# Two downs ahead of the next up at MLP group boundaries, routing two chunks earlier, and no wait behind each of the last slot writes

## The chip, the cores and the metric

The kernel runs on one core of a Trainium2 chip. The metric is the device time of one execution in microseconds, lower is better. Five engines take part: PE (TensorE, the matmuls), DVE (VectorE), ACT (ScalarE), POOL (GpSimd) and SP (SyncE, which only issues DMAs here). Each runs its own instruction list in order, and they meet only at semaphores.

## The reference, cut to what matters

```
scores = scale * q @ k.T, masked to a window of 64      # 4 batches, 8 heads, 576 x 64
x = softmax(scores) @ v                                 # becomes 2304 tokens x 512
h = x @ w_in                                            # 512 -> 2048
x = (h * sigmoid(1.702 * h)) @ w_out                    # 2048 -> 512, the MLP
noisy = x @ w_gate + log1p(exp(x @ w_noise)) * noise    # 8 experts
top2 experts per token, weights = softmax of their two logits
for each expert e: out[tokens of e] += weight * (relu(x @ w1[e]) @ w2[e])   # 512 -> 1024 -> 512
```

## The kernel before, in words

Every fp32 product is made of three fp32r matmuls (high x high, low x high, high x low), so each operand is first split into a high part (ACT, sometimes POOL) and a low part (the rest, by a subtraction on DVE or POOL).

There are three stages: the attention; the MLP; the expert stage, in which tokens lie sorted by expert in a DRAM tensor `x_by_expert` and are worked off in slot tiles of 128 rows.

**The MLP** handles 6 groups (g) of 384 tokens. A group has 16 chunks (c) of the hidden size. On PE an *up* (L1209, 12 matmuls of 384 columns) makes the hidden values of a chunk, and a *down* (L1224, 9 matmuls of 512 columns) adds the chunk to the three accumulators of the group. The down of a chunk stands two places behind its up: up(c), down(c-2). At a group's boundary the order on PE is therefore up(15), down(13), up(0) of the next group, down(14), up(1), down(15), up(2), down(0).

- Between them stand, per chunk: the sigmoid (ACT, L736), its product with the hidden values (DVE, L982), the high part (ACT, L700, `high_of_gate`) and the low part (DVE, L900, `low_of_gate`). In loop step c the two engines do sigmoid and product of chunk c and high and low part of chunk c-1.
- `split_x` makes the high and low parts of the next group's input: four copies on ACT (L695) and four subtractions on DVE (L895). It can start when up(15) has ended, since there is one buffer `xs`. up(0) needs it.
- `copy_y` takes the finished accumulators of a group into `x2` (ACT, L707, two tiles; DVE, L907, one). down(0) of the next group needs the accumulators free. There is one `x2`, so `copy_y` of group g also waits until the scatter of group g-1 has landed:

```
act.wait_ge(accumulated, g * FC + FC)
after(act, x2_turned, g * GT)
after(act, x2_scattered, g * KT * 16)
```

- Routing of group g is threaded through the chunks of group g+1: `turn_x2` and `logits` on PE, `soften`, `choose`, `assign`, `weigh`, `place` on DVE. `place` (last line L967) gives the rows to which tokens go, and then POOL can issue `scatter_x2(g)`, six indirect DMAs (L560) from `x2` to `x_by_expert`.

**POOL during the MLP** splits the expert weights: 128 jobs of two instructions each (L530 high part, L532 low part). Four jobs are a *quad*, so there are 32 quads. SP loads the raw weights and stores both parts. POOL's order is written out by hand: QUADS quads, then for each of the groups 1 to 5 GQUADS quads followed by the scatter of the group before. With QUADS = 2, GQUADS is 6. POOL takes its list in order, so a scatter never starts ahead of the quads in front of it, and a quad never ahead of a scatter that waits.

**The expert stage** takes two ups and a down of 24 matmuls each per slot tile (L1308, L1319: `expert_up` of a tile, then `expert_down` of the tile before). Behind it DVE adds the weighted result to the rows so far (`finish`, L1079), which POOL has gathered from `out` (L599, `gather_part`), and POOL scatters the sum to `out` (L606, `scatter_y`). A gather waits for the writes of earlier experts through a table `settled`; rows of one expert are all different. Tiles from number 35 on are written out one by one, and each of these first waits for its own write before POOL goes on (L634, L640). In this profile 40 tiles run, numbers 0 to 39, and number 35 is the last whose gather waits for an earlier expert.

Of the kernel before, what the change touches and what calls it, by code (L numbers as in the profile page):

```python
# [6 lines left out]
I32 = mybir.dt.int32  # L7
ALU = mybir.AluOpType
# [3 lines left out]
P = 128  # L12
# [28 lines left out]
QUADS = 2  # L41
# [10 lines left out]
FAR = 1 << 16  # L52
LG = 2 * E
# [9 lines left out]
def build(nc, q, k, v, w_in, w_out, w_gate, w_noise, noise, w1, w2, out):  # L63
# [13 lines left out]
    with ctx:  # L77
# [73 lines left out]
        count_to = sbc("count_to", [P, SLOTS])  # L151
        slot_row = sbc("slot_row", [P, SLOTS])
        upto = sbc("upto", [P, E, E], mybir.dt.bfloat16)
        odd = sbc("odd", [P, SLOTS + 1])
# [11 lines left out]
        expert_of = sbc("expert_of", [P, SLOTS], I32)  # L166
        row_of = sbc("row_of", [P, SLOTS], I32)
        ends = sbc("ends", [P, E], I32)
        rows = sbc("rows", [P, SLOTS], I32)
        slot_w = sbc("slot_w", [P, SLOTS])  # L170
        keep = sbc("keep", [P, SLOTS], I32)
        far = sbc("far", [P, SLOTS], I32)
        masked_id = sbc("masked_id", [P, SLOTS], I32)
        passed = sbc("passed", [P, SLOTS, E])
        stepped = sbc("stepped", [P, SLOTS, E])
        past = sbc("past", [P, SLOTS])
        row_f = sbc("row_f", [P, SLOTS])
        first_row = sbc("first_row", [P, SLOTS])
        first_slot = sbc("first_slot", [P, SLOTS])
        settled = sbc("settled", [P, SLOTS], I32)  # L180
        end_row = sbc("end_row", [P, SLOTS])
        valid = sbc("valid", [P, SLOTS])
# [294 lines left out]
        def _(pool):  # L477
# [97 lines left out]
            nc.gpsimd.iota(count_to[:], [[1, SLOTS]], base=0, channel_multiplier=0, allow_small_or_imprecise_dtypes=True).then_inc(slot_consts, 1)  # L575
            nc.gpsimd.iota(slot_row[:], [[P, SLOTS]], base=P, channel_multiplier=0, allow_small_or_imprecise_dtypes=True).then_inc(slot_consts, 1)
            nc.gpsimd.iota(odd[:].rearrange("p (a b) -> p a b", b=2), [[0, (SLOTS + 1) // 2], [1, 2]], base=0, channel_multiplier=0, allow_small_or_imprecise_dtypes=True).then_inc(slot_consts, 1)
# [50 lines left out]
            for j in range(SURE - 1, SLOTS):  # L628
                par = j % 2
                if j < SURE:  # L630
                    gather_part(j, par)
                    scatter_y(j, par)
                    for i in range(2):
                        pool.wait_ge(y_scattered[i], SURE // 2 * 16)  # L634
                else:
                    with pool.If(tiles1 > j + 1):
                        gather_part(j, par)
                        scatter_y(j, par)

                        pool.wait_ge(y_scattered[par], (j // 2 + 1) * 16)  # L640

        @block.scalar
        def _(act):
# [83 lines left out]
            def mlp(g, first):  # L727
                split_x(g)
# [644 lines left out]
```

## Time and profile before

| | us |
|---|---|
| median of 3 runs (lowest, highest) | 1124.26 (1120.97, 1127.78) |
| time of the profiled execution | 1117.89 |
| its span, from first to last instruction | 1116.2 |
| PE busy | 998.9, 89% of the span |
| POOL busy | 528.3, 47% |
| MLP, first up to the end of the last down | 164.0 to 597.8 |
| expert stage, first up to the end of the last down | 642.8 to 1098.5 |

In a timeline a row gives start, length, engine, source line, operation, output and inputs, and in square brackets how long the engine had been idle before it and what ended that. Matmuls of one block are merged into one row; the length of such a row overlaps the next by some 0.16 us, so a block is best measured from its start to the start of the next. A clock of 1.00 is TensorE at 2.4 GHz, 0.50 at 1.2 GHz.

### The profile page before, as it was taken

To read this page: it belongs to the slowest core of one execution; us is meant where nothing else is said; L and a number is where in the kernel's file an instruction comes from. 1 tells how busy PE (TensorE), PEld (TensorE's weight loads), DVE (VectorE), ACT (ScalarE), POOL (GpSimd) and SP (SyncE) were. 2 spreads that over 40 slices of the span, in tenths; PEclk is the share of its full clock that TensorE was granted. 3 is DMA by queue.
4 is the path that set the end of the run, shared out by engine and by line. 5 is a ranking of instruction groups with operands and counts; after the bars stand their busy time and mean duration, and the time that the engine had idled before them with its cause. 6 is when DMAs were issued, how large, how long until landed. Compare 5 with 4: busy or idle time off the path is not lost.

```text
span 1116.2 us, 21003 instructions
## 1 busy us (share of the span) xinstructions
PE 998.9 (89%) x5376; PEld 851.4 (76%) x5377; DVE 628.7 (56%) x1413; ACT 448.6 (40%) x1088; POOL 528.3 (47%) x511
## 2 busy tenths in 40 slices
PE   5777769999999999999996099999999999999993
PEld 5666659879899898898995078888887888888882
DVE  3777752342433527437353467676767676767671
ACT  4877762222424324233242034343443434343440
POOL 3555553896198889898985202121212121212121
PEclk8999989999999999999997599999999999999997
DMA  7678748998189799898888884586858585859211
GB/s 159 166 186 188 184 118 299 289 292 265 40 262 284 253 287 292 270 295 287 265 269 290 279 260 141 183 252 179 255 168 252 169 258 170 266 166 268 65 58 33
DMA packets 253444, 241.65 MB, mean 216 GB/s; under 512 B 97740, under 2 KB 171468, under 8 KB 253392
## 3 DMA queue, kind: packets, MB, share of 16 engines
q1 hardware_dynamic: 215312, 201.54, 60.4%
q0 software_dynamic: 9280, 28.62, 7.2%
q10 hardware_dynamic: 28800, 10.83, 4.3%
q8 instruction: 29, 0.48, 0.2%
q14 instruction: 23, 0.19, 0.1%
HBM read 148.81 MB, written 94.21 MB: 218 GB/s over the span
## 4 chain that ended last, share of the span: by engine, by line
PE 33%; DMA 17%; issue 13%; DVE 11%; ACT 9%; POOL 7%; ACTq 5%; DVEq 2%; POOLq 1%; SPq 1%
PE bank L1209 14%; PE bank L1224 13%; DMA part<-out,yrow 10%; ACT hq L783 4%; DMA out<-y_sb,yrow 4%; ACTq L766 3%; POOL raw L532 2%; ACT he L790 2%; POOL xT L530 2%; DVE y_sb L1079 2%; DMA w_raw<-moe_w_out 1%; PE bank L1244 1%; DVE hT L1067 1%; PE bank L1146 1%; DVEq L1041 1%
## 5 line engine op out<-in xcount | busy, mean ns | idle before, releaser
L1308 PE MATMUL bank<-W,xe 128*128 x960 | 233.2, 399 | 23.5 <-DVE xe L1054 23.5
L1319 PE MATMUL bank<-W,he 128*128 x960 | 230.5, 395 | 4.1 <-DVE he L1071 4.1
L1308 PEld LDWEIGHTS bank<-W,xe 128*128 128x128 f32 x960 | 182.1, 190 | 67.9 <-issue 23.6
L1209 PE MATMUL bank<-xs,W 128*128 128x384 f32 x1152 | 219.8, 340 | 8.7 <-DVE xs L895 8.6
L1224 PE MATMUL bank<-W,gs 128*128 128x512 f32 x864 | 217.1, 396 | 1.0 <-DVE gs L900 1.0
L1319 PEld LDWEIGHTS bank<-W,he 128*128 128x128 f32 x960 | 179.9, 188 | 49.0 <-issue 5.8
L1209 PEld LDWEIGHTS bank<-xs,W 128*128 128x128 f32 x1152 | 200.3, 189 | 17.0 <-issue 10.3
L1224 PEld LDWEIGHTS bank<-W,gs 128*128 128x128 f32 x864 | 161.7, 188 | 31.9 <-DVE gs L900 1.4
L982 DVE TENSOR_TENSOR gate<-bank,gate 128x384 f32<-128x384 f32 x96 | 53.4, 557 | 232.6 <-ACT gate L736 226.2
L606 POOL DMA_INDIRECT out<-y_sb,yrow x40 | 40.6, 1015 | 291.5 <-DVE y_sb L1079 286.1
L783 ACT ACTIVATE hq<-bank 32x256 f32<-32x256 f32 x320 | 119.7, 374 | 112.7 <-issue 99.9
L736 ACT ACTIVATE gate<-bank 128x384 f32<-128x384 f32 x96 | 47.2, 492 | 281.6 <-PE bank L1209 275.0
L1065 DVE STREAM_TRANSPOSE hT<-bank 32x256 f32<-32x256 f32 x320 | 144.0, 450 | 11.2 <-PE bank L1308 6.2
L532 POOL TENSOR_TENSOR raw<-raw,xT 128x512 fp32r<-128x512 f32 x96 | 129.7, 1351 | 7.5
L530 POOL TENSOR_TENSOR xT<-raw,e_iota 128x512 fp32r<-128x512 f32 x96 | 107.0, 1115 | 38.4 <-DMA raw<-moe_w 37.1
L900 DVE TENSOR_TENSOR gs<-gate,gs 128x384 fp32r<-128x384 f32 x96 | 85.1, 888 | 0.0
L773 ACT ACTIVATE xe<-xr 128x512 fp32r<-128x512 f32 x40 | 25.3, 632 | 139.4 <-DVE xr L1050 136.7
L509 POOL TENSOR_TENSOR prob<-prob,rden 128x384 f32<-128x384 f32 x48 | 39.8, 829 | 74.2 <-DVE rden L852 74.2
L1071 DVE SCALAR_TENSOR_TENSOR he<-hT,he 128x1024 fp32r<-128x1024 f32 x40 | 49.0, 1226 | 45.1 <-ACT he L790 45.1
L661 ACT ACTIVATE prob<-prob,nmx 128x128 f32<-128x128 f32 x144 | 56.1, 391 | 27.8 <-DVE nmx L845 27.6
L560 POOL DMA_INDIRECT x_by_expert<-x,xT x36 | 36.9, 1024 | 58.0 <-issue 37.5
L599 POOL DMA_INDIRECT part<-out,yrow x40 | 42.0, 1050 | 34.9 <-POOL yrow L596 34.9
(148 smaller groups left out, 1031.8 us busy)
## 6 DMA issues: line engine op xcount, KB each, us to landing
W<-split_weights SPq DMA_DIRECT2D x128, 512.0 KB
raw<-moe_w SPq DMA_DIRECT2D x128, 256.0 KB, 3.4
split_weights<-raw SPq DMA_DIRECT2D x128, 256.0 KB, 3.3
split_weights<-xT SPq DMA_DIRECT2D x96, 256.0 KB, 3.1
xg<-x_by_expert ACTq DMA_DIRECT2D x160, 64.0 KB
split_weights<-high SPq DMA_DIRECT2D x32, 256.0 KB
q_raw<-q SPq DMA_DIRECT2D x32, 144.0 KB, 2.9
k_raw<-k SPq DMA_DIRECT2D x32, 144.0 KB, 3.9
```

Of the source, the lines that this page charges most:

```text
L530: nc.gpsimd.tensor_tensor(high[buf], job_raw[buf], one, ALU.mult).then_inc(ej_high, 1)
L532: nc.gpsimd.tensor_tensor(job_raw[buf].bitcast(F32R), job_raw[buf], high[buf].bitcast(F32), ALU.subtract).then_inc(ej_low, 1)
L661: ins = nc.scalar.activation(prob[m % 3][:, b], prob[m % 3][:, b], ACT.Exp, bias=nmx[:, m % 2, b:b + 1], accum_out=den[:, m % 2, b:b + 1])
L783: ins = nc.scalar.activation(hq[c * Q:(c + 1) * Q, :].rearrange("p (k q i) -> p k q i", q=2, i=Q)[:, :, q], src[q * Q:(q + 1) * Q, :, c], ...
L900: nc.vector.tensor_tensor(gs[c % 2][:, 1], gate[c % 2][:], gs[c % 2][:, 0].bitcast(F32), ALU.subtract).then_inc(g_low, 1)
L982: nc.vector.tensor_tensor(gate[c % 2][:], h_ps[c % 2][:, 0:TG], gate[c % 2][:], ALU.mult).then_inc(gated, 1)
L1065: nc.vector.transpose(dst[c * Q:(c + 1) * Q, :, q], src[q * Q:(q + 1) * Q, :, c])
L1071: nc.vector.scalar_tensor_tensor(out=he[par][:, 1], in0=hT[:], scalar=0.0, in1=he[par][:, 0].bitcast(F32), op0=ALU.max, op1=ALU.subtract). ...
L1209: ins = nc.tensor.matmul(h_ps[c % 2][:, 0:TG], w_in_s[:, wl, d, c * P:(c + 1) * P], xs[:, xl, d], start=(d == 0 and wl + xl == 0), stop=(d ...
L1224: ins = nc.tensor.matmul(y_ps[t][:], gs[c % 2][:, gl, t * P:(t + 1) * P], w_out_s[:, wl, c], start=(c == 0 and gl + wl == 0), stop=(c == F ...
L1308: ins = nc.tensor.matmul(h2_ps[par][:, f * 512:(f + 1) * 512], xe[par][:, xl, d * P:(d + 1) * P], weights(e, wl, d * FE + f * 512), start= ...
L1319: ins = nc.tensor.matmul(ye_ps[par][:], he[par][:, hl, c * P:(c + 1) * P], weights(e, wl, W1COLS + c * DM), start=(c == 0 and wl + hl == 0 ...
```

## The change

Four things change.

1. At the five group boundaries PE has two downs between up(15) and the next up(0), and two ups behind down(15). ACT and DVE make the parts of chunk 15 right behind `split_x` instead of in step 0.
2. All routing of the group before stands earlier: the copies of the accumulators in step 1 instead of 2, everything after it two steps earlier (`place` in step 12 instead of 14).
3. QUADS is 7 instead of 2, so GQUADS is 5 instead of 6. Ahead of the first scatter POOL has 12 quads instead of 8; ahead of the second 17 instead of 14, then 22 instead of 20, 27 instead of 26, and 32 as before.
4. The slot tables have two more columns; at the very end POOL waits for the number of writes that these hold. The waits behind each single write of tiles 35 and up go.

```
-QUADS = 2
+QUADS = 7
 GQUADS = (EJOBS // 2 - QUADS) // (NG - 1)
+TABLE = SLOTS + 2
...
                 if j < SURE:
                     gather_part(j, par)
                     scatter_y(j, par)
-                    for i in range(2):
-                        pool.wait_ge(y_scattered[i], SURE // 2 * 16)
                 else:
                     with pool.If(tiles1 > j + 1):
                         gather_part(j, par)
                         scatter_y(j, par)
-
-                        pool.wait_ge(y_scattered[par], (j // 2 + 1) * 16)
+            for i in range(2):
+                written = pool.value_load(settled[0:1, SLOTS + i:SLOTS + i + 1], min_val=SURE // 2 * 16, max_val=SLOTS * 16)
+                pool.wait_ge(y_scattered[i], written)
+                pool.sem_inc(wait_passed, 1)
...
@@ ACT @@
             def mlp(g, first):
                 split_x(g)
+                if not first:
+                    high_of_gate(g * FC - 1, FC - 1)
                 for c in range(FC):
                     n = g * FC + c
-                    if c == 2 and not first:
+                    if c == 1 and not first:
                         copy_y(g - 1, 0)
                         copy_y(g - 1, 2)
...
-                    if not (first and c == 0):
-                        high_of_gate(n - 1, (c - 1) % FC)
+                    if c:
+                        high_of_gate(n - 1, c - 1)
...
@@ DVE @@
             def mlp(g, first):
                 split_x(g)
+                if not first:
+                    low_of_gate(g * FC - 1, FC - 1)
...
-                        if c == 14:
+                        if c == 12:
                             place(g - 1)
...
@@ PE @@
             def mlp(g, first):
                 for c in range(FC):
                     n = g * FC + c
+                    if c == 0 and not first:
+                        down(n - 2, FC - 2, g - 1)
                     up(g, c, n)
-                    if not (first and c < 2):
-                        down(n - 2, (c - 2) % FC, g if c >= 2 else g - 1)
+                    if c == 0 and not first:
+                        down(n - 1, FC - 1, g - 1)
+                    if c >= 2:
+                        down(n - 2, c - 2, g)
```

On PE, at the boundary from group 0 to group 1, the order before is (bank<-xs,W is an up, bank<-W,gs a down; the first row is down(12)):

```order
150 L1224 MATMUL bank<-W,gs 128x512 x9
151 L1209 MATMUL bank<-xs,W 128x384 x12
152 L1224 MATMUL bank<-W,gs 128x512 x9
153 L1209 MATMUL bank<-xs,W 128x384 x12
154 L1224 MATMUL bank<-W,gs 128x512 x9
155 L1209 MATMUL bank<-xs,W 128x384 x12
156 L1224 MATMUL bank<-W,gs 128x512 x9
157 L1209 MATMUL bank<-xs,W 128x384 x12
158 L1224 MATMUL bank<-W,gs 128x512 x9
```

and with the change (x18 are two downs, x24 two ups, lines moved by 5):

```order
150 L1229 MATMUL bank<-W,gs 128x512 x9
151 L1214 MATMUL bank<-xs,W 128x384 x12
152 L1229 MATMUL bank<-W,gs 128x512 x18
153 L1214 MATMUL bank<-xs,W 128x384 x12
154 L1229 MATMUL bank<-W,gs 128x512 x9
155 L1214 MATMUL bank<-xs,W 128x384 x24
156 L1229 MATMUL bank<-W,gs 128x512 x9
```

down(14) has moved ahead of up(0), and down(15) ahead of up(1); the transpose of the finished group (bank<-ident,x) follows at once behind the last row, where before three more ups and downs lay between.

On DVE, at the same boundary, before (xs<-xT,xs are the four subtractions of `split_x`, gs<-gate,gs a low part, gate<-bank,gate a product, x<-bank the copy of an accumulator):

```order
178 L900 TENSOR_TENSOR gs<-gate,gs 128x384
179 L895 TENSOR_TENSOR xs<-xT,xs 128x384 x4
180 L975 MEMSET xT 128x4
181 L982 TENSOR_TENSOR gate<-bank,gate 128x384
182 L900 TENSOR_TENSOR gs<-gate,gs 128x384
183 L982 TENSOR_TENSOR gate<-bank,gate 128x384
184 L900 TENSOR_TENSOR gs<-gate,gs 128x384
185 L907 COPY x<-bank 128x4x4x32
```

and with the change:

```order
178 L903 TENSOR_TENSOR gs<-gate,gs 128x384
179 L898 TENSOR_TENSOR xs<-xT,xs 128x384 x4
180 L903 TENSOR_TENSOR gs<-gate,gs 128x384
181 L980 MEMSET xT 128x4
182 L987 TENSOR_TENSOR gate<-bank,gate 128x384
183 L910 COPY x<-bank 128x4x4x32
184 L987 TENSOR_TENSOR gate<-bank,gate 128x384
185 L903 TENSOR_TENSOR gs<-gate,gs 128x384
```

The low part of chunk 15 now stands right behind `split_x`, and the accumulator copy stands ahead of product and low part of chunks 1 and 0. On ACT the two copies likewise stand ahead of the sigmoid of chunk 1.

On POOL, the rows around the first scatter before (raw<-raw is the second instruction of a job; rows 71 to 84 are one quad, run 6 times):

```order
68 L532 TENSOR_TENSOR raw<-raw,high 128x512
69 L569 UNCONDITIONAL_BRANCH
70 L569 ISA
71 L530 TENSOR_TENSOR xT<-raw,e_iota 128x4x128
...
84 L569 COMPARE_AND_BRANCH
85 L560 DMA x_by_expert<-x,xT 19456x528 x6
```

and with the change (rows 111 to 124, run 5 times):

```order
108 L533 TENSOR_TENSOR raw<-raw,high 128x512
109 L570 UNCONDITIONAL_BRANCH
110 L570 ISA
111 L531 TENSOR_TENSOR xT<-raw,e_iota 128x4x128
...
124 L570 COMPARE_AND_BRANCH
125 L561 DMA x_by_expert<-x,xT 19456x528 x6
```

Forty more instructions, five quads, stand ahead of the loop, and the loop runs once less.

## Rows read from the trace of the kernel before

**Rows 1.** The page, busy time of each engine: us, share of the span, instructions.
```profile
PE 998.9 (89%) x5376; PEld 851.4 (76%) x5377; DVE 628.7 (56%) x1413; ACT 448.6 (40%) x1088; POOL 528.3 (47%) x511
```

**Rows 2.** Timeline of PE, boundary of groups 0 and 1: start, us, what, idle before.
```profile
224.66 2.26 PE L1224 MATMUL bank<-W,gs 128*128 128x512 f32 x9
228.99 1.28 PE L1209 MATMUL bank<-xs,W 128*128 128x384 f32 x6 [2.08 <-DVE xs L895]
...
242.08 2.26 PE L1224 MATMUL bank<-W,gs 128*128 128x512 f32 x9
```

**Rows 3.** Timeline of PE, boundary of groups 1 and 2.
```profile
300.61 2.26 PE L1224 MATMUL bank<-W,gs 128*128 128x512 f32 x9
...
313.50 2.26 PE L1224 MATMUL bank<-W,gs 128*128 128x512 f32 x9
```

**Rows 4.** Timeline of PE, down(13) and next down(0) at the three later boundaries.
```profile
372.03 2.26 PE L1224 MATMUL bank<-W,gs 128*128 128x512 f32 x9
...
385.75 2.26 PE L1224 MATMUL bank<-W,gs 128*128 128x512 f32 x9
...
444.28 2.26 PE L1224 MATMUL bank<-W,gs 128*128 128x512 f32 x9
...
458.67 2.26 PE L1224 MATMUL bank<-W,gs 128*128 128x512 f32 x9
...
517.20 2.34 PE L1224 MATMUL bank<-W,gs 128*128 128x512 f32 x9
...
531.71 2.26 PE L1224 MATMUL bank<-W,gs 128*128 128x512 f32 x9
```

**Rows 5.** Timeline of DVE, first boundary and second boundary.
```profile
225.86 1.45 DVE L900 TENSOR_TENSOR gs<-gate,gs 128x384 fp32r<-128x384 f32 x1
227.23 4.95 DVE L895 TENSOR_TENSOR xs<-xT,xs 128x384 fp32r<-128x384 f32 x4
...
302.27 1.96 DVE L895 TENSOR_TENSOR xs<-xT,xs 128x384 fp32r<-128x384 f32 x4
```

**Rows 6.** Timeline of POOL: last job, first scatter, first job and fifth quad after it.
```profile
270.72 1.30 POOL L532 TENSOR_TENSOR raw<-raw,high 128x512 fp32r<-128x512 f32 x1
300.11 1.16 POOL L560 DMA_INDIRECT x_by_expert<-x,xT  x1 [28.09 <-issue]
...
308.00 1.07 POOL L530 TENSOR_TENSOR xT<-raw,e_iota 128x512 fp32r<-128x512 f32 x1
...
351.36 1.04 POOL L530 TENSOR_TENSOR xT<-raw,e_iota 128x512 fp32r<-128x512 f32 x1 [0.59 <-DMA raw<-moe_w]
```

**Rows 7.** Timelines of POOL and ACT: third scatter, and the copies that waited for it.
```profile
447.74 1.15 POOL L560 DMA_INDIRECT x_by_expert<-x,xT  x1 [0.15 <-issue]
...
457.32 1.09 ACT L707 ACTIVATE x<-bank 128x512 f32<-128x512 f32 x2 [1.74 <-DMA x_by_expert<-x,xT]
```

**Rows 8.** Timelines of PE and DVE, the end of the MLP.
```profile
590.25 2.26 PE L1224 MATMUL bank<-W,gs 128*128 128x512 f32 x9
...
607.76 1.97 PE L1237 MATMUL bank<-ident,x 128*128 128x128 f32 x8 [9.82 <-ACT x L707]
...
615.65 0.18 DVE L920 COPY xT<-bank 128x24 f32<-128x24 f32 x1 [8.11 <-PE bank L1244]
```

**Rows 9.** The chain that ended last: the first expert up after the long idle.
```profile
642.76 7.85 PE bank L1308 x24
```

**Rows 10.** Timeline of PE: a later expert up.
```profile
663.47 5.78 PE L1308 MATMUL bank<-W,xe 128*128 x24
```

**Rows 11.** Windows: us, busy of PE, PEld, DVE, ACT, POOL, PE clock, DMA share, GB/s.
```profile
607.00:610.00 3.00, 2.23 (x10) 2.00 (x11) 0.54 (x1) 1.91 (x4) 0.00 (x0) 0.50 0.74 193
...
644.00:646.00 2.00, 2.00 (x6) 1.51 (x6) 0.90 (x3) 0.18 (x1) 0.00 (x0) 0.50 0.99 359
```

**Rows 12.** The chain that ended last, in the tail: start, us, what.
```profile
1094.86 3.94 DMA out<-y_sb,yrow
...
1100.91 3.39 DMA part<-out,yrow
```

More of the change, by code:

```diff
@@ L165, in build @@
         hT = sbc("hT", [P, FE])
-        expert_of = sbc("expert_of", [P, SLOTS], I32)
-        row_of = sbc("row_of", [P, SLOTS], I32)
+        expert_of = sbc("expert_of", [P, TABLE], I32)
+        row_of = sbc("row_of", [P, TABLE], I32)
         ends = sbc("ends", [P, E], I32)
[L169 to L182, printed above, removed]
+        rows = sbc("rows", [P, TABLE], I32)
+        slot_w = sbc("slot_w", [P, TABLE])
+        keep = sbc("keep", [P, TABLE], I32)
+        far = sbc("far", [P, TABLE], I32)
+        masked_id = sbc("masked_id", [P, TABLE], I32)
+        passed = sbc("passed", [P, TABLE, E])
+        stepped = sbc("stepped", [P, TABLE, E])
+        past = sbc("past", [P, TABLE])
+        row_f = sbc("row_f", [P, TABLE])
+        first_row = sbc("first_row", [P, TABLE])
+        first_slot = sbc("first_slot", [P, TABLE])
+        settled = sbc("settled", [P, TABLE], I32)
+        end_row = sbc("end_row", [P, TABLE])
+        valid = sbc("valid", [P, TABLE])
         arenas = [[xT[:, d, TG:2 * TG], TG, 0] for d in range(2)]
@@ L746, in mlp @@
                         nc.scalar.preload_act_table(ACT.Sigmoid)
-                    if c == 12 and not first:
+                    if c == 10 and not first:
                         nc.scalar.preload_act_table_set("natural_log_exp_and_others")
@@ L977, in mlp @@
                     n = g * FC + c
-                    if c == 2 and not first:
+                    if c == 1 and not first:
                         copy_y(g - 1)
@@ L982, in mlp @@
                     nc.vector.tensor_tensor(gate[c % 2][:], h_ps[c % 2][:, 0:TG], gate[c % 2][:], ALU.mult).then_inc(gated, 1)
[L983 to L984 removed]
+                    if c:
+                        low_of_gate(n - 1, c - 1)
                     if not first:
+                        if c == 7:
+                            soften(g - 1)
                         if c == 9:
[L987 removed]
+                            choose(g - 1)
+                        if c == 10:
+                            assign(g - 1)
                         if c == 11:
[L989 removed]
+                            weigh(g - 1)
                         if c == 12:
[L991 to L994 removed]
                             place(g - 1)
```

45 lines of the change are left out of this document (19 added, 26 removed).

## The prediction

> **What bounds the kernel now.** The page comes first: PE is busy for 89% of the span [rows 1], so a change counts where PE stands still or where its clock is low. The chain that ended last gives the places. Through the MLP it runs over ups and downs without a break except at the group boundaries; then come the end of the MLP, the way into the expert stage, and a tail of alternating scatters and gathers. I read each place in the timelines of PE, DVE, ACT and POOL.
>
> - *Boundaries.* From the start of down(13), which is the end of up(15), to down(0) of the next group lie three downs and three ups. This takes 242.08 - 224.66 = 17.42 us at the first [rows 2], 12.89 at the second [rows 3], then 13.72, 14.39 and 14.51 [rows 4]. The second is nearly work alone. The difference is DVE: the four subtractions of `split_x` take 4.95 us at the first boundary, while POOL splits weights, and 1.96 at the second, while POOL issues scatters [rows 5, 6].
> - *POOL.* It finishes its eighth quad at 272.02 and idles 28.09 us until the first routing is placed, then scatters from 300.11 to 308.00 [rows 6]. The later scatters begin with little or no idle [rows 7]. So in this kernel scatters lie right on the boundaries and keep DVE free there.
> - *End of the MLP.* up(15) of the last group ends at 590.25. PE then idles 9.82 us before the transposes, because the copies into `x2` wait for the scatter of group 4, which stands behind the last quad [rows 8].
> - *Tail.* The last gather starts at 1100.91 because it waits for the write started at 1094.86 [rows 12].
>
> **The change, part by part.** Times are of the profiled execution, 1117.89 us, which lies 6.4 us under the median of 1124.26. I forecast a difference and add it to the median.
>
> *1. The first scatter comes late.* This is the term that decides. Twelve quads now stand ahead of it. Eight end at 272.02 (270.72 + 1.30). Four more take 351.36 - 308.00 = 43.4 us [rows 6], so POOL gets to the scatter at 315.4, though its routing is ready before 300. A scatter's first issue lies 9.6 us ahead of the copies that wait for its landing (457.32 - 447.74, rows 7): 315.6 + 9.6 gives 325.2. The accumulators of group 1 are finished by about 310, and down(0) of group 2 can't overwrite them before they are copied. Queued behind the waiting copies are, on ACT, the sigmoid of chunk 1, and on DVE its product and the low part of chunk 0, which down(0) needs too. The copies' 1.09 us [rows 7], about 0.5 each for sigmoid and product (estimates from the rows of the same step), and a low part of up to 1.45 [rows 5] make 3.4 us: down(0) at 328.6. Before, it started at 313.50 [rows 3]. Lag: **+15.1 us**, whatever the first boundary gave. From below: a quad's eight instructions at 1.04 to 1.30 us each [rows 6] make 9.4 us without any wait, four 37.6, and the lag 9.3. From above, with a slower landing and quad, 18.
>
> *2. The clock after the gap.* PE stands still for some 15 us. After the long idle ahead of the expert stage the first up took 7.85 us, a later one 5.78 [rows 9, 10], at a granted clock of 0.50, that is 1.2 GHz [rows 11]. **+2.1 us**; bounds 0 and 3.
>
> The Trainium skill ("TensorE: Matmul & The Clock Gate", What's actually happening) says the throttled clock is the default and activity releases it. The rows at 644 and 663 agree. By it this term is paid once per long gap; without it the sum would be 2.1 lower.
>
> *3. The later boundaries.* The new order gives `split_x` two downs of cover instead of one. But two needs come nearer: down(14) now needs the low part of chunk 14, and down(15) the low part of chunk 15 behind `split_x`. And the routing, two chunks earlier, moves the scatters: `place` ends some 10 us ahead of up(15)'s end, the 7.9 us of scatter issues (308.00 - 300.11) are over by then, and POOL is splitting weights just when DVE splits the input. So each boundary sees DVE as slow as the first did. Counted from up(15)'s end: the low part of chunk 14 starts after 1.20 (225.86 - 224.66) and takes 0.5 to 1.45; `split_x` ends 4.95 later, at 6.7 to 7.6; up(0) ends 0.6 behind it; the low part of chunk 15 delays down(15) by up to 0.9 more; then a down and two ups of 2.1 each, and up to 0.6 for the low part of chunk 0. That is 14.2 to 15.9; I take 14.9. With DVE free it would be 12.9 as in rows 3. At boundaries three to five: 3 x 14.9 - (13.72 + 14.39 + 14.51) = **+2.1 us**; bounds -4 and +5. The first boundary gains 2.5, but that only lengthens the wait of term 1.
>
> The Trainium skill ("SBUF — State Buffer", SBUF: two separate sides) says that VectorE and GpSimd take a shared port pair by an exclusive lock, and the loser is blocked for the whole instruction of the other. It speaks against this change. Here 4.95 against 1.96 us agrees with it. By the rule alone the term would be 3 x 15.9 - 42.62 = +5.1; with no such lock -4.
>
> *4. The end of the MLP.* POOL now fills its 28 us of idle with work, so it has quads left for 500 us only and waits for routing from the third scatter on. The scatter of group 4 lands when up(15) of group 5 ends. Then three downs (6.3 us) and 0.2, and the copies start: 6.5 us behind up(15). PE has not stood still, so the transposes and logits run at 1.00 instead of 0.50 (first window of rows 11). I count 5.2 us from the copies to the last logits: copy 0.9, two transposes, ACT's moves, three logits of 0.8. Before, from 590.25 to 615.65 were 25.4 us [rows 8]; now 11.7: **-13.7 us**. Bounds: -10 with the clock still low, -14.5. The expert weights start to load when the hidden values are all there, still ahead of the first expert up by more than they need, since about 24 us of routing and loads follow unchanged.
>
> *5. The tail.* The gather of tile 39 no longer waits for the write of tile 38 (same expert, other rows). It can be issued some 2 us behind that write's 1.0 us of issue, at about 1097.5, and land after 3.39 us [rows 12] at 1100.9 instead of 1104.3: **-3.4 us**. The last down ends at 1098.5, so the gain is at most 5.8; if the gather queues behind the write it is nothing. The waits of tiles 36 to 38 lie beside PE's work and give nothing. The final wait reads two values while the last write flies: 0. Two more columns in the tables: 0.1.
>
> Sum: 15.1 + 2.1 + 2.1 - 13.7 - 3.4 = **+2.2 us**, 1120.1 for an execution like the profiled one, **1126.5 us** against the median.
>
> **Rivals.**
>
> *A. The quads run faster and the boundaries stay free.* For it: the four quads without DVE or DMA waits need 37.6 us, and POOL's stops for routing could fall on a boundary. Against: 43 us in every stretch of four. Term 1 becomes 15.1 - 5 = 10, term 3 -4: the sum is 10 + 2.1 - 4 - 13.7 - 3.4 = -9.0, or 1115.3.
>
> *B. Thin boundaries throttle PE; slower.* At the first boundary PE stood still for 2.08 us [rows 2] and again twice, and it cost 17.4 us. If each of the three later boundaries costs that, waiting at down(14), up(0) and down(15) in turn until the clock falls as it does after long gaps [rows 11], term 3 is 3 x 17.42 - 42.62 = +9.6: the sum is +9.7, or 1134.0. For it: DVE is in the same contention. Against: the first wait is now shorter, spread over three places, and the third to fifth boundaries cost 13.7 to 14.5 [rows 4]. It decides from 16.1 us per boundary on, where the sum reaches 5.6.
>
> *C. The tail keeps its length.* The gather lands behind the write anyway: 0 instead of -3.4, sum +5.6, or 1129.9.
>
> *D. The gap doesn't open:* the change does what its words say and the scatter is in time. Then terms 1 and 2 are at most -0.5 and the sum -15.5, 1108.8. POOL's order makes this almost impossible, as even 37.6 us for four quads come too late.
>
> **How the numbers follow.** Forecast 0.48, A 0.15, B 0.22, C 0.13, D 0.02. Half a per cent is 5.6 us, about what a measurement of this kernel can tell from no change. Slower by more: B, half of C, 0.04 of the forecast's own spread: 0.33. Faster by more: A, D and 0.02: 0.17, as A needs both its parts, less 0.02 of it. The rest, 0.50, is no change. The forecast's own range is 1121 to 1131; with A and B 1116 to 1136.
>
> **What would show it.** In the profile after: PE idle of about 15 us near 313 to 329, ended by the copies' engines and they by the DMA of the first scatter; a granted clock of 0.50 right behind it; POOL without idle at 272 and with some 10 us each ahead of the later scatters; `split_x` on DVE at 4 to 5 us at all boundaries; PE's idle ahead of the last transposes under 1.5 us and at 1.00; the last gather issued before the last down ends. I am wrong if the first scatter starts before 305, or if `split_x` takes 2 us at the later boundaries.

## The result, and the profile after

The changed kernel takes 1137.43 us (median of 4 runs, 1132.83 to 1139.48). The kernel before, run beside it, takes 1122.62 (4 runs, 1120.88 to 1127.78). The ratio is 1.0119, with a 95% interval of 1.0069 to 1.0169: slower, by 0.7 to 1.7%. A second measurement of the same changed kernel (e5 below) gave 1.0072 [1.0043, 1.0101]. The change costs some 8 to 13 us where 2.2 were forecast. Here and below a median is of all runs, while a ratio leaves out the few that lie more than 1.5% above the fastest of their kernel (one in e5, three in e7).

The profiled execution has a span of 1134.0 us against 1116.2. I cut both spans at the same instructions. A "boundary" runs from the start of down(13), which is the end of up(15), to down(0) of the next group, as in the prediction:

| stretch, us | before | after | difference |
|---|---|---|---|
| attention, up to the first up of the MLP | 163.99 | 166.16 | +2.2 |
| group 0, first up to down(13) | 60.67 | 62.62 | +2.0 |
| first boundary | 17.42 | 15.55 | -1.9 |
| second boundary | 12.89 | 29.37 | +16.5 |
| group 2, down(0) to down(13) | 58.53 | 61.13 | +2.6 |
| third to fifth boundary | 42.62 | 50.35 | +7.7 |
| last down(13) to the end of the logits | 25.37 | 11.79 | -13.6 |
| from there to the first expert up | 27.15 | 27.93 | +0.8 |
| expert stage, to its last down | 449.88 | 455.74 | +5.9 |
| last down and tail | 23.57 | 19.06 | -4.5 |

The groups left out differ by under 0.2 us together. The rows that the change bears on add up to -1.9 + 16.5 + 2.6 + 7.7 - 13.6 + 0.8 - 4.5 = **+7.6 us**. The other three (attention, group 0, expert stage), +10.1 together, are taken up under e5.

**The gap.** The timeline of PE in the changed kernel at the second boundary, which answers to [rows 3]: start, us, what, and in brackets the idle before and what ended it.

```profile
302.92 4.51 PE L1229 MATMUL bank<-W,gs 128*128 128x512 f32 x18
...
309.50 0.79 PE L1214 MATMUL bank<-xs,W 128*128 128x384 f32 x3 [0.76 <-DVE xs L898]
310.81 0.80 PE L1214 MATMUL bank<-xs,W 128*128 128x384 f32 x3 [0.53 <-DVE xs L898]
312.36 2.37 PE L1229 MATMUL bank<-W,gs 128*128 128x512 f32 x9 [0.75 <-DVE gs L903]
...
332.28 4.21 PE L1229 MATMUL bank<-W,gs 128*128 128x512 f32 x9 [13.39 <-DVE gs L903]
```

The releaser named in the last row is DVE's low part, but that is only the end of the chain. One has to follow it back. POOL ends its twelfth quad and issues the first scatter at once:

```profile
318.03 1.28 POOL L533 TENSOR_TENSOR raw<-raw,high 128x512 fp32r<-128x512 f32 x1
319.48 1.16 POOL L561 DMA_INDIRECT x_by_expert<-x,xT  x1 [0.17 <-issue]
```

where before it had idled for 28.09 us and issued at 300.11 [rows 6]. The copies on ACT and DVE wait for that scatter's landing, and sigmoid and low part stand behind them:

```profile
328.92 1.08 ACT L708 ACTIVATE x<-bank 128x512 f32<-128x512 f32 x2 [16.78 <-DMA x_by_expert<-x,xT]
329.89 0.50 ACT L739 ACTIVATE gate<-bank 128x384 f32<-128x384 f32 x1
```

```profile
328.94 0.69 DVE L910 COPY x<-bank 128x512 f32<-128x512 f32 x1 [16.16 <-DMA x_by_expert<-x,xT]
330.90 1.33 DVE L903 TENSOR_TENSOR gs<-gate,gs 128x384 fp32r<-128x384 f32 x1
```

The copies start 9.44 us behind the first issue, as at the third scatter before (9.58, [rows 7]). Counted from down(13), down(0) starts at 332.28 - 302.92 = 29.36 us.

**The clock behind it.** Windows of the changed kernel (columns as in [rows 11]: PE clock third from the end; a value between 0.50 and 1.00 is the mean of a window in which the clock changed from one level to the other):

```profile
332.00:334.00 2.00, 1.72 (x4) 1.44 (x5) 1.38 (x3) 0.90 (x2) 1.92 (x2) 0.50 0.92 275
334.00:336.00 2.00, 2.00 (x6) 1.54 (x6) 0.90 (x1) 0.00 (x0) 1.92 (x3) 0.50 0.98 289
...
402.00:404.00 2.00, 1.23 (x4) 0.83 (x3) 1.45 (x2) 0.49 (x1) 1.92 (x3) 0.63 0.97 316
...
478.00:480.00 2.00, 1.54 (x5) 0.95 (x4) 1.37 (x2) 0.49 (x1) 1.92 (x3) 0.50 0.97 307
...
555.00:557.00 2.00, 2.00 (x11) 1.63 (x10) 0.03 (x1) 0.03 (x1) 1.92 (x3) 1.00 0.96 341
```

The first two lines show the price of the gap (the 2.6 us in the row of group 2). The next two lie inside the third and the fourth boundary, where PE never stood still for longer than 0.8 us at a time, and yet falls to 1.2 GHz. At the fifth (last line) it does not.

**The later boundaries.** DVE at the third boundary, which answers to [rows 5]: `split_x` and the low part of chunk 15.

```profile
395.61 5.82 DVE L898 TENSOR_TENSOR xs<-xT,xs 128x384 fp32r<-128x384 f32 x4
401.36 1.63 DVE L903 TENSOR_TENSOR gs<-gate,gs 128x384 fp32r<-128x384 f32 x1
```

The four subtractions take 5.82 us at all five boundaries, where they took 4.95, 1.96, 2.00, 3.02 and 1.95 before. On PE this gives at the third boundary, beside [rows 4]:

```profile
393.41 4.70 PE L1229 MATMUL bank<-W,gs 128*128 128x512 f32 x18
...
403.04 3.67 PE L1229 MATMUL bank<-W,gs 128*128 128x512 f32 x9 [0.77 <-DVE gs L903]
410.71 2.26 PE L1229 MATMUL bank<-W,gs 128*128 128x512 f32 x9
```

Nine matmuls of a down take 3.67 us instead of 2.26. POOL is what DVE meets. It issued this boundary's scatter from 384.38 on, was back at its weights while up(15) still ran, and split weights beside the four subtractions (last two rows):

```profile
384.38 1.01 POOL L561 DMA_INDIRECT x_by_expert<-x,xT  x1 [3.81 <-DVE xT L970]
...
391.82 1.07 POOL L531 TENSOR_TENSOR xT<-raw,e_iota 128x512 fp32r<-128x512 f32 x1
...
396.79 1.36 POOL L531 TENSOR_TENSOR xT<-raw,e_iota 128x512 fp32r<-128x512 f32 x1
398.23 1.48 POOL L533 TENSOR_TENSOR raw<-raw,xT 128x512 fp32r<-128x512 f32 x1
```

POOL pays too: the same two instructions take 1.04 and 1.30 us when DVE leaves it alone. Ready routing, not a full buffer, let it go: POOL had idled 3.81 us for `place`.

**The end of the MLP and the tail.** PE at the end of the MLP, which answers to [rows 8]: three downs in one row, and the transposes 0.69 us behind them instead of 9.82.

```profile
619.47 6.46 PE L1229 MATMUL bank<-W,gs 128*128 128x512 f32 x27
626.61 1.09 PE L1242 MATMUL bank<-ident,x 128*128 128x128 f32 x8 [0.69 <-ACT x L708]
```

Eight transposes take 1.09 us, not 1.97. In the tail, beside [rows 12], the write of tile 38 is issued at 1117.15 and the last gather right behind it, at 1119.26, before the last down (1114.93 to 1120.80) has ended:

```profile
1117.15 1.02 POOL L607 DMA_INDIRECT out<-y_sb,yrow  x1 [8.40 <-issue]
1119.26 1.05 POOL L600 DMA_INDIRECT part<-out,yrow  x1 [0.88 <-POOL yrow L597]
1124.27 1.01 POOL L607 DMA_INDIRECT out<-y_sb,yrow  x1 [3.97 <-DVE y_sb L1084]
```

### The profile page after: what moved, and what is told of

Its sections match the earlier page's. It is cut to its first block, busy times and chain, and to the rows that moved or that the text cites. A ratio compares the mean times of both kernels' runs of the same rounds, so it can differ in the third digit from the quotient of the medians.

```text
span 1134.0 us, 20971 instructions
## 1 busy us (share of the span) xinstructions
PE 1010.5 (89%) x5376; PEld 854.5 (75%) x5377; DVE 632.9 (56%) x1413; ACT 449.2 (40%) x1088; POOL 528.9 (47%) x511
## 4 chain that ended last, share of the span: by engine, by line
PE 40%; DMA 16%; issue 10%; POOL 9%; DVE 9%; ACT 7%; ACTq 4%; SPq 2%; DVEq 2%; POOLq 1%
PE bank L1229 11%; PE bank L1214 11%; DMA part<-out,yrow 6%; PE bank L1317 6%; PE bank L1328 6%; ACT hq L786 3%; POOL raw L533 3%; DMA out<-y_sb,yrow 3%; POOL xT L531 3%; DMA raw<-moe_w 2%; ACTq L769 2%; DVE xs L898 2%; ACT he L793 2%; DMA w_raw<-moe_w_out 1%; PE bank L1151 1%
## 5 line engine op out<-in xcount | busy, mean ns | idle before, releaser
L1229 PE MATMUL bank<-W,gs 128*128 128x512 f32 x864 | 221.7, 402 | 16.9 <-DVE gs L903 16.6
L1214 PE MATMUL bank<-xs,W 128*128 128x384 f32 x1152 | 223.6, 342 | 8.1 <-DVE xs L898 8.1
L531 POOL TENSOR_TENSOR xT<-raw,e_iota 128x512 fp32r<-128x512 f32 x96 | 107.1, 1116 | 41.2 <-DMA raw<-moe_w 40.4
```

The source lines that it names most:

```text
L531: nc.gpsimd.tensor_tensor(high[buf], job_raw[buf], one, ALU.mult).then_inc(ej_high, 1)
L1214: ins = nc.tensor.matmul(h_ps[c % 2][:, 0:TG], w_in_s[:, wl, d, c * P:(c + 1) * P], xs[:, xl, d], start=(d == 0 and wl + xl == 0), stop=(d ...
L1229: ins = nc.tensor.matmul(y_ps[t][:], gs[c % 2][:, gl, t * P:(t + 1) * P], w_out_s[:, wl, c], start=(c == 0 and gl + wl == 0), stop=(c == F ...
```

## The experiments

My theory at this point: the late first scatter makes the gap (through QUADS = 7); and at the other boundaries it is POOL's weight jobs beside `split_x` that cost, because the earlier routing moved the scatters, which had kept POOL away, ahead of up(15)'s end. Rivals: the new order itself costs at the boundaries (low parts in series with `split_x`); the regrouped jobs are what costs everywhere; the tail gains nothing. Nine kernels were run, and the changed one again. Those in e1 to e4, e5 to e8, and e9 and e10 each shared their runs of the kernel before, with medians of 1122.43, 1120.71 and 1121.71 us.

### e1: the regrouping alone

The kernel before with one line changed.

```
-QUADS = 2
+QUADS = 7
```

> The kernel before with QUADS = 7 and nothing else. Theory (POOL comes too late to the first scatter): the first scatter starts near 320 us instead of 300, PE idles 15 to 17 us ahead of down(0) of group 2 and then runs at clock 0.50 for some 4 us; the later boundaries stay as in the kernel before, since place is still in step 14 and the scatters still cover them; the end of the MLP gains 4 to 6 us. Sum about +13 us, 1136. Rival (the loss comes from the new order on PE, not from the regrouping): within 3 us of the kernel before.

Measured: 1128.38 us (6 runs), 1.0057 [1.0023, 1.0091]. The first scatter starts at 314.15 and the second boundary takes 22.03 us. PE in e1 there:

```profile
324.43 4.18 PE L1224 MATMUL bank<-W,gs 128*128 128x512 f32 x9 [3.69 <-ACT x L707]
```

So the regrouping alone makes this boundary 9.1 us longer, less than was expected of it. Not all of that is the wait for the scatter: PE waits 3.69 us ahead of down(0), and `split_x` takes 5.79 us here too, since no scatter keeps POOL away now. The first boundary, with 5.80 and no scatter to wait for, takes 19.14.

The new order makes the second boundary 7.3 us longer still. Of these, 4.8 are the scatter's place (16.56 us behind down(13) in the changed kernel, 319.48 - 302.92, and 11.75 in e1, 314.15 - 302.40), and 2.5 what stands behind the copies (from the first issue to down(0) 12.80 us against 10.28). Of the 4.8, 3.6 are there because the first boundary is shorter (15.55 against 19.14) and POOL no faster; the other 1.2 did not come back in e5, where the scatter stands 14.60 us behind down(13) (315.22 - 300.62). At the third to fifth boundary e1 takes 12.88 us each, with `split_x` at 1.96. There its scatters start 0.6 to 0.7 us ahead of up(15)'s end (384.9 against 385.5, 456.3 against 457.0, 527.7 against 528.4), and the regrouping costs nothing. The end of the MLP takes 20.67 instead of 25.37.

### e2: the new order without the regrouping

The changed kernel with one line changed back.

```
-QUADS = 7
+QUADS = 2
```

> The changed kernel with QUADS = 2 as before. Theory: no gap at the second boundary, the first scatter near 288 us; but the scatters now end ahead of each boundary, so split_x takes 4 to 5 us on DVE at all five and each boundary lasts 15 to 17.3 us (before 12.9 to 14.5 at the last four). Sum from the terms measured: -1.9 + 2.7 + 3.6 + 2.7 + 1.5 at the boundaries, -12.8 at the end of the MLP, -4.5 in the tail: -8.7, 1114. Rival (two downs cover the split fully): boundaries of 12.6, sum -25. Rival (new order costs as much as it gave in the changed kernel whatever POOL does): above 1130.

Measured: 1116.30 us (7 runs), 0.9947 [0.9920, 0.9975], so the remainder of the change gains. The gap is gone (second boundary 16.29 us, so the late scatter was 13.1 of the changed kernel's 29.37), the end stays at 11.79. Yet all boundaries now take 15.4 to 17.6 us with `split_x` at 5.82, though each had two downs of cover. POOL in e2:

```profile
287.73 1.16 POOL L561 DMA_INDIRECT x_by_expert<-x,xT  x1 [20.25 <-issue]
...
295.29 1.07 POOL L531 TENSOR_TENSOR xT<-raw,e_iota 128x512 fp32r<-128x512 f32 x1
```

The scatter comes 12.4 us earlier than in the kernel before and is over before up(15) ends. This tells the two parts of the change apart: the gap is QUADS, the dearer later boundaries are the earlier routing.

### e3: the tail alone

The MLP of the kernel before on all engines, with the longer tables and without the waits behind each write.

```
-                    for i in range(2):
-                        pool.wait_ge(y_scattered[i], SURE // 2 * 16)
...
-                        pool.wait_ge(y_scattered[par], (j // 2 + 1) * 16)
```

> The kernel before with the longer slot tables and without the waits behind the last writes, MLP untouched. Theory: the last gather starts some 2.1 us behind the last but one write, and the time from the start of the last down to the end of the span falls from 23.6 to about 19.1 us: -4.5, 1118. Rival (the tail gain in the changed kernel was chance): 23 us, no change.

Measured: 1116.81 us (7 runs), 0.9949 [0.9921, 0.9976]. The tail takes 19.13 us, not 23.57. Its last POOL rows show the gather issued 2.11 us behind the write:

```profile
1097.78 1.02 POOL L607 DMA_INDIRECT out<-y_sb,yrow  x1 [8.20 <-issue]
1099.89 1.04 POOL L600 DMA_INDIRECT part<-out,yrow  x1 [0.88 <-POOL yrow L597]
```

The gain of 4.4 us between the two profiles lies within the interval of the ratio (2.7 to 8.9 us). Rival C has fallen. The MLP, which is that of the kernel before, took 19.07 us at its first boundary and 16.59 at its fourth, where the first profile has 17.42 and 14.39: a single boundary can differ by 2 us between executions of one order.

### e4: POOL held back at the later boundaries

If POOL beside `split_x` is what costs, then making POOL wait until DVE is through gives the boundaries back. The changed kernel, with this behind the scatter:

```
                 scatter_x2(g - 1)
+                if 2 <= g < NG - 1:
+                    pool.wait_ge(xs_low, (g + 2) * DC)
+                    pool.wait_ge(g_low, (g + 1) * FC)
```

> The changed kernel, but POOL holds its next quads after the scatters of groups 1, 2 and 3 until DVE has split the next input and made the low part of chunk 15. Theory (DVE is slow at the boundary only because POOL splits weights then): split_x takes 2 us there, the third to fifth boundaries last 12.5 to 13.3 us instead of 17.3, 17.1 and 16.0, the clock stays at 1.00; sum -11 against the changed kernel, 1126. POOL has 10 to 15 us of idle in these groups, so the hold costs nothing. Rival (the boundary is bound by the needs of the new order itself): 16 to 17 us again, 1137.

Measured: 1116.03 us (10 runs), 0.9962 [0.9939, 0.9985], against 1.0119 and 1.0072 without the hold. The third to fifth boundary take 13.02, 13.03 and 13.02 us, the second still 28.55. DVE, PE and POOL in e4 at the third:

```profile
389.04 1.96 DVE L901 TENSOR_TENSOR xs<-xT,xs 128x384 fp32r<-128x384 f32 x4
```

```profile
387.38 4.36 PE L1232 MATMUL bank<-W,gs 128*128 128x512 f32 x18
391.57 2.25 PE L1217 MATMUL bank<-xs,W 128*128 128x384 f32 x12
393.66 2.26 PE L1232 MATMUL bank<-W,gs 128*128 128x512 f32 x9
395.75 4.32 PE L1217 MATMUL bank<-xs,W 128*128 128x384 f32 x24
400.40 2.37 PE L1232 MATMUL bank<-W,gs 128*128 128x512 f32 x9 [0.32 <-DVE gs L906]
```

```profile
391.78 1.04 POOL L531 TENSOR_TENSOR xT<-raw,e_iota 128x512 fp32r<-128x512 f32 x1 [5.65 <-DVE gs L906]
```

POOL stands for 5.65 us, `split_x` takes 1.96 instead of 5.82, and PE has one wait of 0.32 us left. The same order of PE, ACT and DVE costs nothing once POOL is away: the rival by which the order itself costs has fallen. It gains nothing either: the old order took 12.88 us at these boundaries in e1, with `split_x` as short. The three boundaries give back 11.3 us (50.35 - 39.08), as expected; the median is 10 us lower than the 1126 expected, of which 5 are the first measurement of the changed kernel, which e5 did not repeat, and 5 I can't assign.

### e5: the changed kernel again

Nothing is edited; it was run for the size of the effect.

> The changed kernel once more, to tell its own terms from what varies between executions. Theory: the terms of the change come back (boundaries of 15.5, 29.4, 17.3, 17.1, 16.0 us within 1 us each, end of the MLP 11.8, tail 19.1), while the attention (166 us in the first profile, 164 before), the clock at the MLP's first ups and the expert stage (455.7 us against 449.9) come out otherwise: from the terms alone +8, 1131. Rival (the slower expert stage belongs to the change): expert stage of 455 to 457 us again and 1137.

Measured: 1130.98 us (median of 10 runs, one of them at 1984.02, which no other run of any kernel resembles), 1.0072 [1.0043, 1.0101]. Its boundaries (15.50, 27.40, 17.12, 16.00, 17.05 us), its end (12.20) and its tail (19.27) are those of the first measurement within 2 us each, where the expectation allowed 1, and its own terms add up to +6.1 us by the same rows as above. This time the fourth boundary is the one without a fall of the clock, at 16.00 us.

What differs between the two is what varies in all kernels. Group 0 takes 60.66 us in six of the ten experiments and in the kernel before, and 62.4 to 63.4 in the other four and in the changed kernel: there the first ups of the MLP run at half clock, as the window in the changed kernel (first) shows, and not in the kernel before (second):

```profile
166.20:168.20 2.00, 2.00 (x6) 2.00 (x7) 1.31 (x3) 1.75 (x3) 0.00 (x0) 0.50 1.02 237
```

```profile
164.00:166.00 2.00, 2.00 (x12) 1.98 (x13) 1.34 (x3) 1.78 (x3) 0.00 (x0) 1.00 1.02 242
```

Attention ends at 159 to 166 us, though no two kernels differ there. The expert stage took 455.0 us again in e5, as the rival had it. But e4 and e7, with the same expert stage, took 449.0 and 450.7, and e1, with the old one, 455.3, so its length doesn't follow the change. Here it is in the kernel before and in the changed one:

```profile
642.80:1092.60 449.80, 445.75 (x1896) 357.52 (x1896) 313.02 (x634) 186.80 (x399) 87.14 (x115) 1.00 0.64 193
```

```profile
659.20:1114.90 455.70, 449.22 (x1896) 359.29 (x1896) 312.83 (x634) 187.19 (x399) 87.73 (x115) 0.99 0.63 192
```

PE does the same 1896 matmuls. It is idle 2.4 us longer (6.5 against 4.1 us), and its busy time is 3.5 us longer at a clock of 0.99 instead of 1.00. There are stalls such as this one of the changed kernel, where DVE waits for a partial result; what makes them longer in one execution than in another I have not traced:

```profile
970.84 0.75 DVE L1084 SCALAR_TENSOR_TENSOR y_sb<-bank,slot_w,part 128x512 f32<-128x512 f32 x1 [2.85 <-DMA part<-out,yrow]
```

I count these 10 us as belonging to single executions. That the change has no part in them is likely from this spread, not shown: there is one profile per measurement, and the two of the changed kernel have nearly the same expert stage.

### e6: the old routing steps in the new PE order

e2, with all that the change had moved earlier on ACT, DVE and PE put two steps later again (the accumulator copies one). In short:

```
-                    if c == 1 and not first:
+                    if c == 2 and not first:
                         copy_y(g - 1, 0)
...
-                        if c == 12:
+                        if c == 14:
                             place(g - 1)
```

> The changed kernel with QUADS = 2 and all routing steps back at the old chunks (place in step 14), so that only the order at the boundaries and the tail are new. Theory: the scatters begin at the boundaries again, split_x takes 2 us at the last four, and these last 12.6 to 13.1 us each; the first 15.5. No gap. The end of the MLP stays at 24 to 25 us, since the scatter of group 4 still follows the last quad. Sum: 72.9 of boundaries before become 67.5, tail -4.5: -10 us, 1112.5. Rival (the new order is slow in itself): boundaries of 15 us or more although split_x takes 2 us.

Measured: 1115.66 us (10 runs), 0.9950 [0.9923, 0.9976]. The boundaries take 16.89, 12.80, 13.20, 13.54 and 13.94 us, with `split_x` at 5.83 at the first and 1.95 to 2.00 at the others, and the end 24.99. So in the new PE order too it depends on the scatter's place how long `split_x` takes; between these two profiles the pair of downs is worth 0.1 to 0.9 us per boundary; and the shorter end comes from the earlier routing. What e6 gains over the kernel before is no more than the tail alone gives in e3, about half of the 10 us expected. Beside e2 it shows what the earlier routing is worth by itself: it takes 13.2 us off the end (24.99 against 11.79) and puts 11.0 on the five boundaries (70.4 against 81.4 in sum).

### e7: early routing, and the scatter put on the boundary by counting quads

If one wants the short end *and* free boundaries, the scatter has to be issued when up(15) ends, not when its routing is ready. e2 with ten quads ahead of the first scatter:

```
+AT = [2, 10, 16, 22, 28, 32]
...
-                with pool.Fori(QUADS + (g - 1) * GQUADS, QUADS + g * GQUADS) as i:
+                with pool.Fori(AT[g - 1], AT[g]) as i:
```

> The changed kernel with the quads ahead of the scatters chosen by time: 10, 16, 22, 28, 32 in sum. Theory (a scatter should start 5 us ahead of to 1 us behind the end of up(15), then it is in time for the copies and keeps POOL off DVE during the split): first scatter near 295 us, no gap, the last four boundaries at 13 us, the first at 15.5, end of the MLP 12 us, tail 19. Sum -5.4 - 13 - 4.5 = -23, 1100. Rival (28 quads are too many, the fourth scatter is late): a gap of 3 to 8 us at the fifth boundary, 1104 to 1108.

Measured: 1112.81 us (12 runs), 0.9892 [0.9852, 0.9932]. The end takes 11.79 us, yet the boundaries take 16.2 to 17.2. The profile shows a near miss at the second boundary: the last issue and the first weight job of POOL, then `split_x` on DVE, all within 1.3 us. The scatters that should cover the second to fifth split start 5.6 to 7.1 us ahead of the end of up(15), where the expectation allowed 5:

```profile
300.59 1.32 POOL L561 DMA_INDIRECT x_by_expert<-x,xT  x1 [0.30 <-issue]
301.92 1.07 POOL L531 TENSOR_TENSOR xT<-raw,e_iota 128x512 fp32r<-128x512 f32 x1
```

```profile
300.98 5.31 DVE L898 TENSOR_TENSOR xs<-xT,xs 128x384 fp32r<-128x384 f32 x4
```

The twelve times fall into two lots, three at 1098.8 to 1102.7 and nine at 1112.3 to 1119.5 us, which fits an edge between "POOL back before `split_x`" and "behind it"; only an execution of the slower lot was profiled.

### e8: nine quads, and a hold ahead of the first boundary

```
-QUADS = 2
-AT = [2, 10, 16, 22, 28, 32]
+QUADS = 3
+AT = [3, 9, 15, 21, 27, 32]
...
+            pool.wait_ge(xs_low, 2 * DC)
+            pool.wait_ge(g_low, FC)
             for g in range(1, NG):
```

> As the kernel with 10, 16, 22, 28, 32 quads, but POOL stops after its third quad until the first boundary's split and low part are done, and the sums are 9, 15, 21, 27, 32. Theory: the first boundary too lasts 13 us, the rest as there: another -2.5, 1097. Rival (POOL has no time to spare for the stop): the scatters slip by up to 10 us and later boundaries or the end of the MLP give it back, 1100 or more.

Measured: 1101.07 us (6 runs), **0.9815 [0.9778, 0.9851]**, the lowest median of all. `split_x` takes 1.96 us at every boundary, these take 12.54, 12.54, 13.57, 14.69 and 13.12, the end 11.79, the tail 19.03. PE at its first boundary, against [rows 2], and POOL beside it:

```profile
225.96 4.36 PE L1231 MATMUL bank<-W,gs 128*128 128x512 f32 x18
230.15 2.25 PE L1216 MATMUL bank<-xs,W 128*128 128x384 f32 x12
232.24 2.26 PE L1231 MATMUL bank<-W,gs 128*128 128x512 f32 x9
234.34 4.33 PE L1216 MATMUL bank<-xs,W 128*128 128x384 f32 x24
238.50 2.26 PE L1231 MATMUL bank<-W,gs 128*128 128x512 f32 x9
```

```profile
230.35 1.04 POOL L531 TENSOR_TENSOR xT<-raw,e_iota 128x512 fp32r<-128x512 f32 x1 [10.87 <-DVE gs L905]
```

There is no gap between any two of the PE rows. POOL's 10.87 us of idle cost nothing at this boundary or the next, since it had 28 us to spare. Later the rival was right in part: the third scatter starts 1.8 us behind the end of up(15) (442.12 against 440.32), PE waits 1.85 us there, and the fourth boundary takes 14.69; the median is 4 us above the 1097 expected.

### e9 and e10: a hold behind each scatter

Does the two-lot behaviour of e7 go once POOL can't come back early? e9 is e7, and e10 is e8 with the third and fourth scatter a quad earlier, each with

```
                 scatter_x2(g - 1)
+                if g < NG - 1:
+                    pool.wait_ge(xs_low, (g + 2) * DC)
+                    pool.wait_ge(g_low, (g + 1) * FC)
```

> The kernel with 10, 16, 22, 28, 32 quads ahead of the scatters, whose runs fell into two groups (1099 to 1103 and 1112 to 1119) and whose profile had scatters that were over before the split; new is only that behind each scatter POOL stops until the next input is split and the low part of chunk 15 is made. Theory (the slow group is the one in which POOL goes back to splitting weights just before DVE's split): split_x 2 us at the last four boundaries, these 12.5 to 14.7 us, the first 15.5 to 17; one group of runs, 1098 to 1105, median 1102. Rival (the two groups come from the expert stage or the attention): still two groups, some 12 us apart.

Measured: e9 takes 1101.55 us (5 runs, 1097.37 to 1105.20), 0.9842 [0.9809, 0.9875], in one lot. Its second to fifth boundaries take 12.5 to 13.1 us with `split_x` at 1.96 each, so the miss in e7 was POOL's return. The rival (two lots from the expert stage or the attention) is unlikely by five runs in one lot, where e7 had nine of twelve in the other.

> As the kernel with sums 9, 15, 21, 27, 32 and one stop at the first boundary, but sums 9, 15, 20, 26, 32 and a stop behind every scatter. Theory: the third scatter, which came 1.8 us behind the end of up(15) there and made that boundary 14.7 us, comes in time; all boundaries 12.5 to 13.1: -2 us, 1099. Rival (the stops and the last six quads make the fifth scatter late): the end of the MLP grows beyond 12 us, 1101 or more.

Measured: e10 takes 1105.90 us (5 runs), 0.9869 [0.9836, 0.9901]. All boundaries are free (12.5 to 13.0), but the end of the MLP takes 19.43 us instead of 11.79. PE there:

```profile
584.21 6.46 PE L1234 MATMUL bank<-W,gs 128*128 128x512 f32 x27
595.79 1.97 PE L1247 MATMUL bank<-ident,x 128*128 128x128 f32 x8 [5.12 <-ACT x L713]
```

The scatter of group 4 starts at 581.4, only 2.8 us ahead of the end of up(15), where e8 has 8.1 (577.3 against 585.4); it lands too late for the copies. e8, e9 and e10 overlap in their times; which of them is best is open.

## Why the prediction came out as it did

The forecast was 1126.5 us, in a range of 1121 to 1131, or 1116 to 1136 with rivals A and B. The first measurement, 1137.43, lies above both; the second, 1130.98, just inside. The outcome with the highest chance, 0.50, was no change, that is less than 5.6 us; by both ratios (13 us, and 8 with an interval from 4.8 on) it is the one that had 0.33, slower. The sum said +2.2 us; the same terms measure +7.6, and +6.1 in e5, nearly all of the difference in one of them. Term by term:

*1. The late first scatter: right.* Forecast: issue at 315.4, lag +15.1 us at down(0) of group 2. Measured: issue at 319.48, and the two boundaries together 14.6 us longer (-1.9 + 16.5). The issue came 4 us later than forecast, of which 4.1 are attention and group 0 of this execution (+2.2 and +2.0). The bracket [9.3, 18] holds it. The four quads took 42.8 us (276.48 to 319.31), where I had 43.4. (The parts of the "3.4 us" behind the copies add up to 3.5; it changes nothing.) e1 and e2 show the cause: QUADS alone makes PE wait for the scatter, and without it there is no such wait.

*2. The clock after the gap: right*, 2.6 us against 2.1.

*3. The later boundaries: the step that failed.* The mechanism was right, the size wrong. I forecast 14.9 us per boundary, +2.1 in all; they took 17.30, 17.05 and 16.00, **+7.7 us**, outside the bounds of -4 and +5. Two things were mis-sized:

- I took the contention of the first boundary (4.95 us for `split_x`) as its full price and allowed the low part 1.45. But there POOL's jobs covered the subtractions only in part: POOL stood still for want of raw weights in the midst of them (row below), and one of the four took 0.55 us. With POOL at work throughout the four take 5.82 us, 1.46 each on average against 0.49 when free, and the low part behind them 1.63. That is about 1.0 us more for each, close to one POOL instruction (1.04 to 1.30 us). In e1 and e3, where the first boundary stands as before, they took 5.80 and that boundary 19.1 us. Down(15) starts 9.6 us behind down(13) (403.04 - 393.41), where the middle of my count had 8.2. (The lower end of the count, with nothing at its two "up to", is 13.6 and not 14.2.) The boundary without a fall of the clock took 16.0 against 14.9.
- The short waits are not free for the clock: at two of the three boundaries it fell, to 0.50 to 0.63 in the windows. These took 17.30 and 17.05 us, the one without 16.00: 1.2 us each more. e5 has the same split, 17.12 and 17.05 against 16.00.

POOL in the kernel before, at its first boundary, beside the subtractions of 227.23 to 232.18 [rows 5]:

```profile
228.91 1.31 POOL L530 TENSOR_TENSOR xT<-raw,e_iota 128x512 fp32r<-128x512 f32 x1 [0.47 <-DMA raw<-moe_w]
```

What came is rival B, with its mechanism (waits at up(0), down(15) and their like in turn, the clock falling) and nearly its price (+9.6 forecast by B, +7.7 measured). I had given it 0.22 because the old later boundaries were cheap. That was the wrong evidence: they were cheap because of the scatters that the change moved away, as term 3 itself said. Experiments e4 and e9 show that POOL's place is the whole of it: the same order with POOL held takes 12.5 to 13.1 us, at a clock of 1.00. Why the clock fell at some of the boundaries with short waits and not at others stays open.

The Trainium skill ("SBUF — State Buffer", SBUF: two separate sides) had the size nearly right: when a VectorE instruction with two SBUF inputs and a GpSimd instruction want the shared port pair, the one that comes second waits for the whole of the other. The mean of 1.46 us for one of the four, against 0.49, agrees with it. The prediction worked out +5.1 by it, without a fall of the clock (three boundaries of 16.00 would be +5.4), and then went by a row of partial contention.

*4. The end of the MLP: right*, -13.6 against -13.7, and the clock at 1.00 in the transposes, as forecast. The way from there to the first expert up changed by 0.8.

*5. The tail: right in kind*, -4.5 against -3.4 (e3: -4.4 alone). The gather went out 2.1 us behind the write, where I had counted 2.6 (1097.5 - 1094.86). The other 0.5 us lies behind the last write's issue: from there to the end are 9.72 us against 10.23, and 9.7 to 9.8 in all runs with the new tail; which part of the end that is I did not trace.

What isn't a failed step is the remaining 10 us between the two profiled executions. The spread of e1 to e10 in attention (159 to 166), group 0 (60.7 or 62.4 to 63.4) and the expert stage (449 to 457) is as large, and the second measurement of the changed kernel came out 5 us lower against the kernel before than the first.

Where the gain of the whole idea was: the end (-13.6), the tail (-4.5) and boundaries with POOL out of the way (66.5 us for all five in e8 against 72.9 before). e8 keeps all of these by other numbers of quads ahead of the scatters and one hold, and is 1.85% [1.49, 2.22] faster than the kernel before.

## What to carry to other kernels

Before you move an instruction stream earlier, look at what it kept *away* by standing where it stood: here six DMA issues on POOL shielded DVE, and moving them cost more than the new order gained. When two engines contend, price the contention from full overlap (here about one instruction of the other for each of yours), not from a row in which they overlapped in part. And if a helper engine has idle time, put it by an explicit wait where the critical engine needs peace, rather than by counting jobs that end close to an edge.

## What was not expected of the hardware

- DVE subtractions of 128x384 fp32 with two SBUF inputs: 1.96 us for four while POOL issues scatters or waits, 5.82 while it runs `tensor_tensor`; DMA issues on POOL don't hold DVE up here, its vector instructions do. POOL's two instructions take 1.36 and 1.48 us meanwhile, instead of 1.04 and 1.30. The product with the hidden values, whose one input comes from PSUM (`gate<-bank,gate`), takes 0.55 us beside POOL at work (at 402.91) as without it.
- The granted clock fell to 0.50 (1.2 GHz) beside waits of 0.46 to 0.77 us only, at two boundaries of the changed kernel (third and fourth), and stayed at 1.00 at two others, with waits of 0.52 to 0.76 us (first and fifth).
- The granted clock was 0.50 in the first microseconds of the MLP in some executions and 1.00 in others, of kernels that don't differ up to there; it is worth 1.7 to 2.7 us.
